# Attention, MoE and gated MLP on one core: raw keys and queries of two heads turned in one transpose, split into parts on the way out of PSUM, and put in place by DMA

## The reference, cut to what matters

```python
def _attn_ref(q, k, v):                     # q, k, v: (4, 8, 1152, 64), float32
    q_pool = q.reshape(B, H, S // 2, 2, D).mean(axis=3)
    scores = (1 / sqrt(D)) * matmul(q_pool, k.transpose(0, 1, 3, 2))
    attn = softmax(scores)
    return matmul(attn, v)                  # (4, 8, 576, 64)

def reference(**kw):
    x = attn_out.transpose(0, 2, 1, 3).reshape(2304, 512)
    x = moe(x)      # top-1 of 8 experts, each 512 -> 1024 -> 512
    return gated_mlp(x)                     # 512 -> 1536 -> 512
```

## Time and profile before

| what | value |
|---|---|
| median of 3 runs | 1524.81 us |
| profiled execution, its own time | 1529.89 us |
| span of that execution | 1527.9 us |
| attention | from 0 to about 655 us of the span |
| PE, DVE, ACT, POOL busy over the whole span | 93%, 56%, 45%, 33% |
| mean granted TensorE clock | 0.975 |

### The profile page before, as it was taken

How to read it: one execution, slowest core, us unless ns; L and a number is a source line. 1 busy time by engine, 2 the same in 40 slices (tenths; PEclk the granted TensorE clock), 3 DMA queues, 4 the chain that set the end, 5 groups by cost and what they waited for, 6 DMA issues and landing times. The chain is left out here.

```text
span 1527.9 us, 25839 instructions
## 1 busy us (share of the span) xinstructions
PE 1425.5 (93%) x8085; PEld 1236.9 (81%) x8086; DVE 854.6 (56%) x1602; ACT 684.4 (45%) x1635; POOL 504.6 (33%) x340
## 2 busy tenths in 40 slices
PE   4999999999999999983997899998999999999998
PEld 3788888888888888762786787886999999999997
DVE  4788777777777778755443444443643232323222
ACT  4878888888888887751214301101521111111111
POOL 2664444444444432047728802203201010110000
PEclk9999999999999999995998999999999999999999
DMA  7421111111111121245626713112521010100000
GB/s 263 127 56 54 54 54 54 54 54 54 54 54 54 54 65 31 75 139 206 221 96 208 245 41 96 55 41 88 157 65 35 7 35 7 34 7 21 0 21 21
DMA packets 87034, 117.00 MB, mean 77 GB/s; under 512 B 8784, under 2 KB 47696, under 8 KB 86992
## 3 DMA queue, kind: packets, MB, share of 16 engines
q1 hardware_dynamic: 71072, 74.50, 15.6%
q10 hardware_dynamic: 12880, 31.99, 6.2%
q0 software_dynamic: 3040, 9.96, 2.0%
HBM read 87.33 MB, written 29.10 MB: 76 GB/s over the span
## 5 line engine op out<-in xcount | busy, mean ns | idle before, releaser
L648 DVE TENSOR_TENSOR p_lo<-ps_t,p_hi 128x512 fp32r<-128x512 f32 (+1 forms) x336 | 221.3, 670 | 81.7 <-ACT p_hi L509 78.5
L509 ACT ACTIVATE p_hi<-ps_t 128x512 fp32r<-128x512 f32 (+1 forms) x336 | 193.0, 585 | 73.8 <-PE ps_t L697 71.8
L573 DVE TENSOR_REDUCE maxima<-ps_s 128x1 f32<-128x512 f32 x288 | 196.6, 683 | 33.0 <-PE ps_s L804 30.8
L1039 POOL TENSOR_TENSOR w_parts<-raw_w,w_parts 128x1024 fp32r<-128x1024 f32 x64 | 150.9, 2394 | 190.4 <-ACT w_parts L1109 190.2
L533 ACT ACTIVATE probs<-ps_s,neg_max 128x512 f32<-128x512 f32 x288 | 199.9, 694 | 15.7 <-DVE neg_max L586 15.6
L697 PE MATMUL ps_t<-ident,probs 128*128 128x128 f32 x1296 | 191.5, 273 | 0.0
L697 PEld LDWEIGHTS ps_t<-ident,probs 128*128 128x128 f32 x1296 | 156.6, 140 | 33.2
L1655 ACT ACTIVATE silu<-ps_g 128x384 f32<-128x384 f32 x72 | 35.4, 491 | 314.8 <-PE ps_g L1761 314.8
L804 PE MATMUL ps_s<-kq_t 128*128 128x512 f32 x512 | 168.1, 410 | 4.9 <-ACT probs L533 3.1
L1109 ACT ACTIVATE w_parts<-raw_w 128x1024 fp32r<-128x1024 f32 x64 | 67.0, 1057 | 222.0 <-PE ps_h L1436 105.0
L1708 DVE TENSOR_TENSOR silu<-ps_g,silu 128x384 f32<-128x384 f32 x72 | 40.1, 557 | 210.3 <-ACT silu L1655 210.2
(11 more groups left out here) (212 smaller groups left out, 3210.8 us busy)
## 6 DMA issues: line engine op xcount, KB each, us to landing
raw_w<-in_moe_w ACTq DMA_DIRECT2D x61, 512.0 KB, 4.1
raw_k<-in_k SPq DMA_DIRECT2D x16, 576.0 KB, 4.0
raw_v<-in_v SPq DMA_DIRECT2D x16, 576.0 KB, 3.8
raw_q<-in_q SPq DMA_DIRECT2D x32, 256.0 KB, 4.0
x_by_slot<-zeros SPq DMA_DIRECT2D x1, 6400.0 KB, 19.5
y_by_slot<-x_out SPq DMA_DIRECT2D x25, 256.0 KB, 2.0
kept_rows<-x_by_slot SPq DMA_DIRECT2D x23, 256.0 KB, 2.7
out<-kept_rows SPq DMA_DIRECT2D x18, 256.0 KB, 2.2
```

What stands on the lines that cost most here:

```text
L509: nc.scalar.activation(p_hi[m % PT][:, 0:w], T[ring(kind, j)][:, 0:w], ACT.Copy).then_inc(hi_ready, 1)
L573: nc.vector.reduce_max(maxima[:, 3 * tile + h:3 * tile + h + 1], S[(2 * tile + h) % SR][:, :], AX).then_inc(max_done, 1)
L648: nc.vector.tensor_tensor(p_lo[m % PT][:, 0:w], t[:, 0:w], p_hi[m % PT][:, 0:w].bitcast(F32), ALU.subtract).then_inc(t_free_dve, 1)
L1039: nc.gpsimd.tensor_tensor(w_part(n, parity, 1, at, PIECE), raw[j % RAW][:, :], w_part(n, parity, 0, at, PIECE).bitcast(F32), ALU.subtract) ...
```

## The change

- Chunks no longer hold two parts of one head, but the raw values of both: a chunk has 64 dimensions of head 0 and beside them 64 of head 1. `raw_k` is loaded by two transfers, one a head, each landing in runs of 64 values; query sums go into a `q_sum` interleaved in the same way. 9 chunks of keys and 5 of queries make 14, turned in 4 groups of 4, 4, 4 and 2.
- The split comes after the turn: ACT writes the first part of a group, scaled, to `parts` (`group_hi`), and DVE the second from the same PSUM bank (`group_lo`, five instructions a pair). `parts` is one buffer of 3584 columns.
- In `parts`, head 0 lies on partitions 0 to 63 and head 1 on 64 to 127. The matmuls need both parts of one head over 128 partitions. SP moves them: `copy_parts`, six SBUF-to-SBUF transfers a pair, three for each head, of 64 rows each with 9728, 4608 and 5120 bytes a row. They go out when DVE has finished group 3. PE waits for all six ahead of the scores of the next pair's tile 0.
- The loads of pair p+2's keys and queries go out behind the copies of pair p+1, as the raw buffers are read by the transposes themselves; POOL then only adds the query rows (`q_sums`). Its splits of keys and queries and the padding are gone.
- The list of steps, now `UNITS`, keeps the order with 5 g's and one x fewer: the last ones are `("g", 3)` at place 22, `("a", 5)`, `("a", 6)`, `("a", 7)`, `("a", 8)`, with the scores of tile 8 at places 22 and 23 and of the next pair's tile 0 at places 25 and 26. The first g stands at place 1, as before.
- ACT and DVE both release T banks through one semaphore, as DVE now reads every bank last. x has two steps of 4 tiles.

```diff
+    GROUP_CHUNKS = [(0, 4), (4, 8), (8, 12), (12, 14)]
-    X_TILES = [(0, 3), (3, 6), (6, 8)]
+    X_TILES = [(0, 4), (4, 8)]
+    UNITS = [
+        ("b", 0), ("g", 0), ("b", 1), ("b", 2), ("b", 3), ("b", 4), ("b", 5), ("b", 6), ("b", 7),
+        ("b", 8), ("g", 1), ("c", 0), ("c", 1), ("c", 2), ("x", 0), ("a", 0), ("a", 1), ("x", 1),
+        ("a", 2), ("g", 2), ("a", 3), ("a", 4), ("g", 3), ("a", 5), ("a", 6), ("a", 7), ("a", 8),
+    ]
+    SCORES_AT = [(25, 26), (0, 1), (3, 4), (6, 7), (11, 12), (14, 15), (17, 18), (21, 21), (22, 23)]
...
+                    for h in range(2):
+                        sp.dma_start(raw_k[:, :].rearrange("p (c h d) -> p c h d", h=2, d=D)[:, :, h, :],
+                                     k_rows[bass.ds(2 * p + h, 1)].rearrange("h p (c d) -> (h p) c d", d=D)
+                                     ).then_inc(kq_loaded, 16)
...
+                def copy_parts(par):
+                    for h in range(2):
+                        src, at = parts[h * D:h * D + D].bitcast(F32), h * HEAD
+                        sp.dma_start(kq_t[par][0:D, at:at + HEAD].bitcast(F32), src[:, 0:LO_K]).then_inc(kq_copied, 16)
+                        sp.dma_start(kq_t[par][D:P, at:at + CH * P].bitcast(F32), src[:, LO_K:LO_K + CH * P]
+                                     ).then_inc(kq_copied, 16)
+                        sp.dma_start(kq_t[par][D:P, at + CH * P:at + HEAD].bitcast(F32), src[:, CH * P:LO_K]
+                                     ).then_inc(kq_copied, 16)
...
+                def next_pair(p, par, kind, load=True):
+                    sp.wait_ge(t_free, upto(p, kind, every, LAST_G))
+                    copy_parts(1 - par)
+                    if load:
+                        load_kq(p + 2)
+                        sp.wait_ge(v_split, p + 2)
+                        load_v(p + 2)
...
-                def split_kq_of(p, par, chain):
-                    rk, rq, qs, kp, qh, ql = split_views(par)
...
+                def q_sums(p):
+                    rq = raw_q[:, :].rearrange("p (t r d) -> p t r d", t=TILES, r=2)
+                    pool.wait_ge(kq_loaded, 16 * KQ_DMAS * (p + 1))
...
+                def group_hi(g, bank):
+                    c0, c1 = GROUP_CHUNKS[g]
+                    nc.scalar.activation(parts[:, c0 * P:c1 * P], T[bank][:, 0:(c1 - c0) * P], ACT.Copy,
+                                         scale=HALF_SCALE).then_inc(kq_hi_done, 1)
...
+                        last = nc.vector.scalar_tensor_tensor(
+                            out=parts[:, at:at + (b - a) * P], in0=T[bank][:, (a - c0) * P:(b - c0) * P],
+                            scalar=HALF_SCALE, in1=parts[:, a * P:b * P].bitcast(F32), op0=ALU.mult,
+                            op1=ALU.subtract)
...
-                        pe.wait_ge(kq_split, p + 2)
-                        last = group(1 - par, i, t)
+                        if i == 0:
+                            pe.wait_ge(kq_loaded, 16 * KQ_DMAS * (p + 2))
+                            pe.wait_ge(q_summed, 2 * (p + 2))
+                        last = group(i, t)
...
+                    if tile == 0 and h == 0:
+                        pe.wait_ge(kq_copied, 16 * COPIES * (p + 1))
```

More of the change, by code:

```diff
@@ L169, in attention @@
     UNIT_LAST = {"a": ("a", CH - 1), "b": ("b", CH - 1), "c": ("c", 2)}
+    LAST_X = ("x", len(X_TILES) - 1)
+    LAST_G = ("g", GROUPS - 1)
+    assert sum(map(is_prob, UNITS)) % PT == 0 and LAG < PT
+    assert UNITS[-LAG:] == [("a", CH - LAG + j) for j in range(LAG)]
     ctx = ExitStack()
@@ L329, in _ @@
                              ).then_inc(ys_zeroed, 16)
[L330 to L338, removed]
+                next_pair(0, 0, "first")
+                with sp.Fori(1, LAST - 2, 2) as p:
+                    next_pair(p, 1, "mid")
+                    store(p - 1, "mid")
+                    next_pair(p + 1, 0, "mid")
+                    store(p, "mid")
+                next_pair(LAST - 2, 1, "mid")
+                store(LAST - 3, "mid")
+                next_pair(LAST - 1, 0, "mid", load=False)
                 w16 = shared.w16[:, :].rearrange("p (c e) -> p c e", e=2 * E)
@@ L411, in split_v_of, with body @@
                                             ).then_inc(v_split, 1)
[L413 to L420, removed]
-                split_v_of(0, 0, 2)
[L425 to L435, removed]
+                q_sums(0)
+                split_v_of(0, 0, 2)
+                pool.wait_ge(t_filled, GROUPS)
+                q_sums(1)
+                def body(p, par, kind, sums=True):
                     if kind != "first":
                         pool.wait_ge(pv_done, upto(p, kind, is_prob, ("c", 2)))
-                    split_v_of(p + 1, 1 - par, chain + 2)
-                    pool.wait_ge(t_free_act, upto(p, kind, by_act, ("g", 8)))
-                    pad(p + 1, 1 - par)
+                    split_v_of(p + 1, 1 - par, 3 + p)
+                    if sums:
+                        pool.wait_ge(t_filled, upto(p, kind, every, LAST_G))
+                        q_sums(p + 2)
                 body(0, 0, "first")
@@ L500, in take @@
                     act.wait_ge(t_filled, before(p, kind, every) + j + 1)
-                    if by_act(step):
-                        group(1 - par, step[1], ring(kind, j))
+                    if is_group(step):
+                        if step[1] == 0:
+                            act.wait_ge(kq_copied, 16 * COPIES * (p + 1))
+                        group_hi(step[1], ring(kind, j))
                         return
@@ L686, in _ @@
-                second_parts(0)
+                    for n, step in enumerate(UNITS):
+                        if step in steps(kind):
+                            take(p, par, kind, j, step)
+                            if lagged(kind, j) in UNIT_LAST.values():
+                                outputs(p, kind, lagged(kind, j)[0])
+                            j += 1
+                        for tile in (*range(1, TILES), 0):
+                            if kind == "tail" or (kind == "last" and tile == 0):
+                                continue
+                            of = p if tile else p + 1
+                            if MAXIMA_AT[tile][0] == n:
+                                largest_half(of, tile, 0)
+                            if MAXIMA_AT[tile][1] == n:
+                                largest_half(of, tile, 1)
+                                largest_rest(of, tile)
@@ L687, in _ @@
+                    if kind == "tail":
+                        for n in range(j, j + LAG):
+                            if lagged(kind, n) in UNIT_LAST.values():
+                                outputs(p, kind, lagged(kind, n)[0])
+                for g in range(GROUPS):
+                    dve.wait_ge(kq_hi_done, g + 1)
+                    group_lo(g, g % TR)
                 largest_half(0, 0, 0)
@@ L806, in scores, with scores_rem @@
                     last.then_inc(s_ready, 1)
-                def scores_rem(p, par, tile, waits=True):
-                    if waits:
+                def scores_rem(p, par, tile, opening=False):
+                    if not (opening and tile == 0):
                         pe.wait_ge(exp_rem_done, TILES * p + tile)
@@ L847, in _ @@
-                pe.wait_ge(consts_ready, 1)
-                pe.wait_ge(kq_split, 1)
+                    for n, step in enumerate(UNITS):
+                        if step in steps(kind):
+                            fill(p, par, kind, j, step)
+                            done = lagged(kind, j)
+                            if done is not None and is_prob(done):
+                                products(p, par, kind, j - LAG, done)
+                            j += 1
+                        for tile in (*range(1, TILES), 0):
+                            if kind == "tail" or (kind == "last" and tile == 0):
+                                continue
+                            of = (p, par) if tile else (p + 1, 1 - par)
+                            opening = kind == "first" and tile > 0
+                            if SCORES_AT[tile][0] == n:
+                                scores(*of, tile, 0, opening)
+                            if SCORES_AT[tile][1] == n:
+                                scores(*of, tile, 1, opening)
+                                if tile % QT == 0:
+                                    scores_rem(*of, tile, opening)
@@ L849, in _ @@
+                    if kind == "tail":
+                        for n in range(j, j + LAG):
+                            if is_prob(lagged(kind, n)):
+                                products(p, par, kind, n - LAG, lagged(kind, n))
+                pe.wait_ge(consts_ready, 2)
+                pe.wait_ge(kq_loaded, 16 * KQ_DMAS)
+                pe.wait_ge(q_summed, 2)
                 for g in range(GROUPS):
                     if g >= TR:
-                        pe.wait_ge(t_free_act, g - TR + 1)
@@ L853, in _ @@
-                    group(0, g, T[g % TR]).then_inc(t_filled, 1)
```

(9 more changed lines are left out.)

289 lines of the change are left out of this document (100 added, 189 removed).

## The result

The changed kernel takes 1721.19 us in the median of 4 runs (1714.06 to 1721.95), the kernel before 1525.79 us (4 runs, 1521.59 to 1527.8): a ratio of 1.1274, 95% interval 1.1236 to 1.1313. The forecast was 1692 us, range 1585 to 1765. The profiled execution has a span of 1719.2 us, 191.3 us over that of before.

What follows compares the result with a forecast made beforehand. PE was taken as the bound, busy 38.1 or 38.2 of 38.9 us a pair. Copy wait +150, loads and clock +46, transposes -31, opening +3 gave +168 on 1529.9: 1698 us, 1692 against the median; range 1585 to 1765.

Steps and rivals of the forecast that it cites:

- The copy's wait: PE's wait ahead of the next pair's tile 0 for the six transfers: 10.0 us, 15 times, +150 us.
- Start: Time from the last g's start until SP issues the copy: 1.6 us.
- PE's need: Time from the last g's start until PE wants the copied data for tile 0: 5.3 us.
- the chosen halving of the 407 GB/s: Copy's data rate taken as half the fastest row's, 204 GB/s: 12.2 us for 2.49 MB a pair.
- The rivals with the full rate: Copy runs at 407 GB/s, wait 3.9 us ahead of tile 0: +62 us, 1587 us; chance 18%.
- a much slower one: Copy much slower than half rate, 97 GB/s at the end: 1895 us, 1790 halfway; chance 10%.
- Loads and clock: Behind the copy, wait for the moved loads and lowered PE clock: 3.3 us together, 14 times, +46 us.
- The transposes saved: PE turns 14 chunks a pair in place of 36: 2.1 us less, over 15 lists 31 us less.
- Both stay under ... so I cost them at nothing: ACT at 28.2 and DVE at 33.4 us a pair stay under PE's 36.8, so their changed work costs nothing.
- The opening: Before the first scores and in the first list: copy lands near 26.1, 3.5 us later; net +3 us.

Runs made afterwards that it cites:

- the wide copy: Changed kernel with 14 of 15 copies moving the same bytes in six transfers over 128 partitions, not between halves (scores wrong): 1639.64 us, one run.
- the half copy: Changed kernel with six 64-partition transfers each moving only half its columns in 14 of 15 transitions (scores wrong): 1639.28 us, one run.
- held two-queue run: Changed kernel with head 0's copies issued by SP, head 1's by ACT, and SP holding the next loads until all six copies landed: 1766.19 us.
- the two runs on the clock and the loads: Each against the changed kernel: 96 identity transposes on PE ahead of the copy wait, 1725.59 us; keys loaded in runs of 2304 bytes, 1717.18 us.
- the early order: Changed kernel with the g steps moved from places 1, 10, 19, 22 to 1, 5, 9, 12: 1540.1 us, ratio 1.0094 to the kernel before.
- the run with the clock held up: Changed kernel with 96 transposes of the identity into the free R bank ahead of PE's wait for the copy: 1725.59 us.
- the keys in one run: Changed kernel with keys loaded as before, one transfer in runs of 2304 bytes (scores wrong): 1717.18 us, one run.

## Why the prediction was right, and where it was off

Point by point, per pair in the steady part, measured against forecast.

- **The copy's wait**: 10.2 to 10.4 against 10.0 us. Start (1.5 against 1.6 us) and PE's need (5.3 us) were as read from the rows; the chosen halving of the 407 GB/s was borne out by the wide and the half copy, and the 14.3 us to landing exceed the 13.7 a little. The rivals with the full rate and with a much slower one are out.
- The rule of the Trainium skill (SBUF — State Buffer, "Door 1: The DMA port swizzle") gives the right size: about 218 GB/s for 64 partitions, 198 by the two copies here. The Trainium skill (DMA: Bandwidth & Descriptors, "Rules for kernel authors") says that two transfers to disjoint halves serialize. The landing of the held two-queue run agrees (14.0 us against 14.3); its 240 GB/s with both halves in flight, against 196 with one, shows that they overlapped a little.
- **Loads and clock**: forecast 3.3 us together, between 2.5 and 4.0, with the larger hiding the smaller. The first g came 7.0 us after the landing where 4.0 of work stand: 3.0. The size is right, and so is the shape, by the two runs on the clock and the loads.
- **The transposes saved**: 2.1 forecast. PE's busy time fell from 38.1 to 36.6 in the early order, 1.5 us; in the run with the clock held up it is 35.9 without the 10.7 us of added transposes, 2.2 us. The rows do not settle it closer.
- **"Both stay under ... so I cost them at nothing"** is a step that failed. DVE's and ACT's sums were right, but PE's short waits behind them grew from at most 0.9 to 1.9 us a pair (0.96 + 0.73 + 0.26). An engine need not be the busiest to be waited for: in the early order a part of that work stood right ahead of the copy of the output bank. Without the copy's wait this alone eats the saving: PE busy 1.5 us less, idle 1.3 us more.
- **The opening**: scores 7.0 us later, not 3.5. The first copy took its usual 14.1 us, but POOL's sums ended at 10.8 us where 8.8 was forecast, and the copy was issued at 15.5. With the keys in one run it was issued at 13.7, so some 2 us of this are the keys' shorter runs. Another 2 us come behind the last pair's first scores. Some 9 us in all where +3 was forecast.

By these rows a pair grows by 10.4 (copy) + 1.2 (sums) + 1.7 (slow clock, PE busy 37.6 against 35.9) + 1.0 (short waits) - 2.2 (transposes) = 12.1 us; measured are 12.2, against 11.2 forecast. In all it is 191 us against 168: the forecast is low by the short waits, the copy's 0.4 and the opening. The term on which most hangs, the halved rate, was a choice between two ends with no row for it; that it came out is partly luck. That the copy could not be covered follows from the forecast's own terms (1.6 + 1.5 + 6.1 us at the full rate against PE's 5.3), and the wide copy bears it out with a wait of 4.8 us and 1639.64 us.

No version tried here beats the kernel before. Whether an order exists that frees PE of the waits for DVE and ACT is open, and so is what the early order would take with a shorter opening.

## What to carry to other kernels

A producer moved from an engine's output to a DMA needs cover as long as issue, flight and data together; count what the consumer still has to do between the last input and the first use before anything else, and if the order is kept, that number decides. And when a reordering has removed the steady waits, compare the openings too: here they held what was left of the difference. Where two delays start at the same event, taking one away shows the other: test both before pricing either. And when the bound engine is relieved by handing work to one at 80%, look at what that work is queued ahead of, not at the busy sum.

## What the runs showed of the hardware

SBUF-to-SBUF transfers of 64 rows moved 205 to 212 GB/s, of 128 rows 404, the latter two at the same row lengths, with the 16 DMA engines shown busy in all of them (0.94 to 1.02). With the two heads issued from two queues the rate was 240 GB/s while both were in flight, and the landing came no earlier. An issue of a copy on SP took 0.5 us when the queue was free and up to 2.55 us behind queued copies. What keys in runs of 256 bytes cost beside 2304 is not told apart from nothing in the whole kernel's time (one run, 4 us less, inside the spread of the changed kernel); in its opening it was 2.0 us.
